# Attention and mixture of experts on one core: on TensorE, the scores of two steps ahead are computed before the last step is turned back, instead of after

## The reference

```
rel = pos[:, None] - pos[None, :]                    # per batch and head
scores = q @ k.T / sqrt(64) + slope[h] * (-abs(rel)) where 0 <= rel < 128, else -1e9
attn = softmax(scores);  x = attn @ v                # x: 2304 tokens x 512 (8 heads x 64)
logits = x @ w_gate                                  # 8 experts
e[i] = argmax(logits[i]);  gate[i] = softmax(logits[i])[e[i]]
# each expert keeps its first `capacity` tokens, in order of token
out[i] = gate[i] * (relu(x[i] @ w1[e[i]]) @ w2[e[i]])  # 512 -> 1024 -> 512, zero where not kept
```

## Time and profile before

| | us |
|---|---|
| median of 3 executions | 483.32 |
| lowest, highest | 481.99, 488.57 |
| the profiled execution | 483.09 |
| its span, first to last instruction | 481.4 |

### The profile page before, as it was taken

How to read it: one execution, slowest core, us unless ns; L and a number is a source line. 1 busy time by engine, 2 the same in 40 slices (tenths; PEclk the granted TensorE clock), 3 DMA queues, 4 the chain that set the end, 5 groups by cost and what they waited for, 6 DMA issues and landing times.

```text
span 481.4 us, 11741 instructions
## 1 busy us (share of the span) xinstructions
PE 440.9 (92%) x2902; PEld 355.3 (74%) x2903; DVE 282.6 (59%) x825; ACT 216.9 (45%) x573; POOL 88.5 (18%) x139
## 2 busy tenths in 40 slices
PE   8798889989988797869999999999999999999992
PEld 7586667757766675438888888888888888888872
DVE  4587567667766978664636666266266666622230
ACT  3676657766767554116144442343244444411110
POOL 5090000000000820031112111111211121111110
PEclk9999899999999977789999999999999999999998
DMA  9945353354467401725616666166166666111110
GB/s 163 237 143 129 88 133 90 90 134 84 117 145 140 179 33 24 185 69 196 219 44 216 218 216 218 43 211 217 31 206 212 205 214 207 44 44 34 44 44 14
DMA packets 78857, 63.53 MB, mean 132 GB/s; under 512 B 61614, under 2 KB 61614, under 8 KB 78832
## 3 DMA queue, kind: packets, MB, share of 16 engines
q1 hardware_dynamic: 75312, 52.47, 39.8%
q0 software_dynamic: 3520, 10.76, 7.1%
HBM read 53.77 MB, written 10.23 MB: 133 GB/s over the span
## 4 chain that ended last, share of the span: by engine, by line
PE 68%; DMA 15%; DVE 6%; SPq 4%; issue 3%; ACT 1%; POOL 0%; DVEq 0%; POOLq 0%
PE ps L1138 48%; DMA k_rows<-in_k 12%; PE ps L1155 4%; PE ps L1023 3%; PE ps L993 3%; PE ps L958 3%; PE ps L980 3%; PE ps L1012 2%; SPq L298 2%; PE ps L1131 2%; DMA x_rows<-x_sb 2%; DVE probs L656 1%; DVE x_sb L688 1%; SPq L315 1%; PE ps L1090 1%
## 5 line engine op out<-in xcount | busy, mean ns | idle before, releaser
L1138 PE MATMUL ps<-weights_sb,rowsT_hi 128*128 (+1 forms) x336 | 106.6, 398 | 0.0
L1138 PE MATMUL ps<-weights_sb,hiddenT_hi 128*128 x336 | 103.5, 389 | 1.2 <-DVE hiddenT_lo L877 1.2
L594 ACT ACTIVATE hidden<-ps 128x512 f32<-128x512 f32 x21 | 12.5, 597 | 147.7 <-PE ps L1138 147.7
L896 DVE TENSOR_TENSOR weights_sb<-raw,weights_sb 128x1024 f32 (+1 forms) x56 | 67.1, 1220 | 16.5 <-issue 9.5
L527 ACT ACTIVATE probs<-probs,mins 128x256 f32<-128x256 f32 (+2 forms) x160 | 73.7, 467 | 0.0
L1138 PEld LDWEIGHTS ps<-weights_sb,hiddenT_hi 128*128 128x128 f32 x336 | 63.0, 188 | 14.5 <-issue 1.4
L1138 PEld LDWEIGHTS ps<-weights_sb,rowsT_hi 128*128 128x128 f32 x336 | 61.8, 189 | 12.5 <-issue 0.6
L1138 PE MATMUL ps<-weights_sb,rowsT_lo 128*128 (+1 forms) x168 | 65.8, 392 | 0.0
L1138 PE MATMUL ps<-weights_sb,hiddenT_lo 128*128 x168 | 65.4, 389 | 0.0
L877 DVE TENSOR_TENSOR hiddenT_lo<-ps,hiddenT_hi 128x512 fp32r<-128x512 f32 x42 | 27.1, 687 | 60.1 <-ACT hiddenT_hi L598 60.1
L583 ACT ACTIVATE weights_sb<-raw 128x1024 f32 (+1 forms) x56 | 56.5, 1065 | 5.5 <-DVE src_row L829 5.5
(11 more groups left out here) (123 smaller groups left out, 535.6 us busy)
## 6 DMA issues: line engine op xcount, KB each, us to landing
raw<-in_moe_w SPq DMA_DIRECT2D x64, 512.0 KB, 4.2
q_rows<-in_q SPq DMA_DIRECT2D x16, 256.0 KB, 3.9
k_rows<-in_k SPq DMA_DIRECT2D x16, 256.0 KB, 4.6
v_rows<-in_v SPq DMA_DIRECT2D x16, 256.0 KB, 5.0
x_rows<-x_sb SPq DMA_DIRECT2D x16, 256.0 KB, 3.2
q_rows<-in_q SPq DMA_DIRECT2D x4, 128.0 KB, 4.5
k_rows<-in_k SPq DMA_DIRECT2D x4, 128.0 KB, 4.7
v_rows<-in_v SPq DMA_DIRECT2D x4, 128.0 KB, 4.7
```

The costliest lines, as they stand in the source:

```text
L896: vec.tensor_tensor(weights_sb[:, slot, 2 * layer + 1, part].rearrange("p s n -> p (s n)"), raw[:, j, :], weights_sb[:, slot, 2 * layer, p ...
L1138: ins = te.matmul(dst, left[a], right[c], start=first and n == 0, stop=last and n == 2)
```

## The change

In each step on TensorE, `score` for the step two ahead moves from behind `turn_back` (and, in the last batch's step 5, from behind the first counts of the routing) to a place ahead of the wait for the copy of q or k and ahead of `turn_back`. In the first batch's step 1 a wait for the gate's weights is added in front of `turn_back`; the same wait ahead of the first batch (line 1106) stays.

```diff
                     turn_probs(b, kk, 0)
                     turn_probs(b, kk, 1)
+                    if not (last and kk + 2 >= STEPS):
+                        score(b + (kk + 2) // STEPS, (kk + 2) % STEPS)
+                    if first and kk == 1:
+                        pe.wait_ge(wg_landed, 48)
                     if not (first and kk == 0):
                         if turns and quad == 0:
                             wait_alone(pe, qT_ready, tb * TI + ti + 1)
                         if turns and quad == 1:
                             wait_alone(pe, kT_ready, tb * TI + ti + 1)
                         turn_back(b + (kk - 1) // STEPS, (kk - 1) % STEPS)
                     if last and kk == 5:
 
                         pe.wait_ge(onehot_ready, 1)
                         own_unit(early_ranks_ps, 0, EARLY, True)
                         add_counts(early_ranks_ps, EARLY, range(EARLY - 1), False, True).then_inc(ranked, 1)
-                    if not (last and kk + 2 >= STEPS):
-                        score(b + (kk + 2) // STEPS, (kk + 2) % STEPS)
                     if last and kk == 5:
                         pe.wait_ge(early_kept, 1)
                     mix(b, kk)
```

## The result

| | before | changed |
|---|---|---|
| median, us | 484.50 (4 runs) | 505.47 (4 runs) |
| lowest, highest | 481.99, 488.57 | 502.90, 506.16 |
| profiled execution, its span | 483.09, 481.4 | 505.57, 503.9 |

The ratio is 1.0415, with a 95% interval of 1.0331 to 1.0499: the change makes the kernel 4.2% slower. Forecast were 497 us and a range of 489.5 to 507. The median before is 1.2 us above the 483.32 of three executions, because a fourth, of 485.67 us, was added.

A forecast was written before the change was run, and what follows sets the result against it. The prediction took the attention stage's loop from round head through turning back, store and load to be the bound. 483.09 + 8.2 + 5.6 (clock falls) = 496.9, given as 497 us; range 489.5 to 507.

The forecast's parts named there:

- The loop of head, turning back, store, load and next head: Attention rounds of tiles 3, 4, 0 and 1: the period is this loop; normalising to next head takes 6.18 us.
- The loop's price: Scores between head and turning back: +8.3 us, less 0.8 in the first batch, left +7.5.
- the terms: Scores less removed waits, in us: tile 2 +0.9, tile 3 +0.8, tile 4 +0.5, tile 0 +0.6, +0.4, +0.7.
- TensorE's clock: Longer waits at heads drop it to 1.2 GHz: four more falls at 1.4 us, 5.6 us, bounds 0 to 16.
- The waits for the copies: TensorE's waits for copies of k (4.5 us) and q (2.0) nearly vanish; some 5 us end up at heads.
- VectorE: Later normalising and bias are covered by idle time: nothing in the first three batches; uncovered, up to 8 us.
- The last batch: VectorE also does the routing there, its cover is thin and the bias comes later: +0.7 us, bounds 0 and 1.5.
- The loop alone: Rival: the loop costs, the clock falls no more than now; 491.3 us, within 490 to 493, chance 0.22.
- Absorption by faster loads: Rival: later loads land faster or have slack, at most 0.5 us in each of twelve; 483 to 489 us, chance 0.10.
- The other side: Rival: loads do not bind at the heads, scores fill the waits for q and k; 477.3 us, chance 0.03.
- A clock low over long stretches: Rival: TensorE's clock stays low, all twelve heads pay 2.0 us; above 507 us, chance 0.05.

The follow-up runs named there:

- The same microsecond of work: The kernel before with 9 transposes of the identity ahead of turning back: ratio 1.0298 in the even steps, 1.0074 in the odd.
- The kernel with the clock held: The changed kernel with 8 to 16 transposes of the identity ahead of q transposes in rounds that wait for a load: 493.49 us, ratio 1.0194.

## Why the prediction was right, and what it mis-sized

**The loop of head, turning back, store, load and next head** is shown. The same microsecond of work costs 14.4 us in the even steps and 3.6 in the odd; with the loads taken out of the loop the 20 us of the new order are gone.

**The loop's price** was 7.5 us to the head of the last batch's tile 1. The kernel with the clock held stands 7.0 behind there, and 8.3 without the fall that the kernel before has. In the nine passages of the changed kernel at full clock the terms add up to 6.5 and the trace has 6.4. That the sum is so close is in part luck, for singly they are less good: tile 2 to 3 was put at 0.9 and took 0.84, 0.74 and 1.29; tile 3 to 4 at 0.8, with 0.38, 0.79 and 0.92; tile 4 to 0 at 0.5, with 0.28 and 0.20; and tile 0 to 1 in the third batch at 0.4, with 1.00.

**TensorE's clock** was the term that was too small, in the right direction: four falls at 1.4 us, 5.6. The kernel that holds the clock is 12 us faster than the changed one (2.2% by the ratios, 10.7 us), of which some 8.4 came with the fills. In the changed kernel's passages with a low stretch, what the loop's terms do not explain is some 10 us: 1.8, 1.3, 1.3, 1.4, 1.4 and 2.5. So it was six passages at 1.6, with five falls, and a sixth fall behind the last of the twelve heads, at 170.74, is in the last batch's time. One passage, 1.8, is the first batch's round of tile 0, behind the very first wait for a load (2.30 us, 1.80 before), where the two kernels have not yet differed: that is chance and not the change. At this place the profiled executions of all fourteen kernels can be compared: the clock held in twelve, after 1.20 to 2.07 us, and fell in two, after 2.30 and 2.31. Four more falls than before, apart from that one, is what was forecast; they cost more, 7.9 us in these passages and 1.6 in the last batch, in place of 5.6. From about 52.5 to 66 us the clock was low without a break, for longer than a whole round, which the estimate of separate falls did not have.

**The waits for the copies** were rightly counted as no saving outside the loop, and the prediction put some 5 us of them into the waits at the heads. In the traces that is what they do: the odd steps' waits, 0.26 to 0.79 us each before, broke the idle time into pieces, and with the odd steps also in the new order it stands in one piece ahead of the head. The clock fell once in the first three batches before, four times with the new order in the odd steps, three times with it in the even ones, and five times with both. These are single executions. The prediction had the new waits about right, twelve of 1.9 us each and 2.4 the longest: between 36 and 172 us the trace has eleven, 19.7 us together and at most 2.5. The twelfth, at 61.19, is filled by TensorE's own slow work.

**VectorE** was costed at nothing in the first three batches. It took 0.9 us in one place, where its operation on the sums ran 1.64 us beside a split of GpSimd (its preparation of the second stage's weights) and the bank was emptied late; five waits of TensorE for the bank are 2.4 us in all, of which 0.7 is in the last batch.

**The last batch** was put at +0.7 and took +3.2. About half of that can be the fall behind its first head, 1.6 us: transposes of the probabilities, scores and turning back take 1.40, 2.08 and 1.03 us there in place of 1.04, 1.13 and 0.73. The trace also has two VectorE operations of the changed kernel that ran long, here with the split beside the first:

```profile
177.36 2.36 POOL L456 TENSOR_TENSOR weights_sb<-raw,weights_sb 128x1024 fp32r<-128x1024 f32 x1
177.96 1.90 DVE L719 SCALAR_TENSOR_TENSOR code<-is_top,iota_eE 128x120 f32<-128x120 f32 x1
...
181.41 1.80 DVE L674 TENSOR_SCALAR sums_eps<-sums 128x8 f32<-128x8 f32 x1
```

They took 0.28 and 0.16 before. Further on the one-hots have three long operations, of 1.36, 1.03 and 2.31 us, where the kernel before has two, of 2.33 and 1.01. Which operations meet a split depends on when the batch starts. That the phase, and not the order, put them there is argued from this and not shown, and the shares of the 3.2 us stay open.

**The rivals.** The loop alone, 491.3, is about what remains when the clock is held (493.5 with all of the rest). Absorption by faster loads did not occur: the page has the loads of 256 KB landing 3.9 us (q) and 4.6 us (k) after their issue in the median, in both kernels. Nor does this agree with the estimate of 2.6 us that the prediction worked out from the Trainium skill, "DMA: Bandwidth & Descriptors", section "Anatomy of one DMA", whose fit is for GpSimd's path and not for the SP queue used here. The other side, with the scores filling the waits, needs the loop open; when it was opened by hand, the new order was not slower, though not faster by 5.8 us either. A clock low over long stretches came once, from 52.5 to 66 us, and not at all twelve heads.

## What to carry to other kernels

Before work is moved forward on the busiest engine, find what the work that it overtakes releases: here a normalising on VectorE and a store on SP's queue stood between the delayed work and a load whose landing set the next round. A wait that fills with useful work gains only if the time does not return as a longer wait elsewhere, and idle time gathered in one place may cost more than the same time in pieces, because TensorE's clock can fall behind it. The remedy was not in the order at all: the loads waited for a store that they had nothing to do with.

## What the runs showed of the hardware

Idle time of TensorE can cost more than itself: with useless transposes in it the changed kernel took 493.5 us in place of 505.5, some 8.4 us of it by the fills. Up to 176 us the granted clock of the changed kernel fell to the level of 1.2 GHz after waits of 1.69 to 2.46 us, six times, and held after six of 1.26 to 1.87; with the new order in the odd steps alone it fell after one of 1.40. With the waits filled it stayed at 2.4 GHz for 120 us.

Some VectorE operations of 0.16 to 0.28 us took up to 2.34 us when they met a GpSimd operation with two inputs, and ended with it: 155.25 and 2.34 us of the one, 155.20 and 2.36 of the other. The Trainium skill, "SBUF — State Buffer", section "SBUF: two separate sides", says that the two share a pair of ports as an exclusive lock held for a whole instruction, where VectorE's operation is in a two-port mode or has two inputs in SBUF. The trace agrees in that the one ends with the other; in which mode these operations ran, no run here shows.
